# Attention tiles: rows and keys turned head by head, gate logits summed in PSUM, and the scalar and vector steps in a new order

## The chip, the core and the metric

The kernel runs on one core of a Trainium2 chip. The metric is the device time of one execution in microseconds. PE is TensorE (PEld its weight loads), DVE is VectorE, ACT ScalarE, POOL GpSimd, SP SyncE. A tile here is 128 tokens; a tile's index is written t, and its place in its batch c = t mod 6.

## What is computed

The reference has three stages. The change touches the first one and its handover to the second.

```python
def _attn_ref(q, k, v, f_logit):          # 4 batches, 8 heads, 768 tokens, 48 channels a head
    f = 1.0 / (1.0 + np.exp(-f_logit))
    for t in range(S):
        state = f[:, :, t, :, None] * state + np.einsum('bhd,bhe->bhde', k[:, :, t], v[:, :, t])
        y[:, :, t] = np.einsum('bhd,bhde->bhe', q[:, :, t], state)
# x = y by token: 3072 x 384; logits = x @ w_gate (8 experts)
# _moe_ref: (token, expert) pairs in falling order of logits, each expert takes N/8 = 384 tokens;
#           out[mask] = relu(x[mask] @ w1[e]) @ w2[e]
# _moe2_ref: g = elu(x @ w_in); g @ w_out
```

## The kernel before

`attention` goes through 24 tiles, six to a batch. Four pairs of heads lie side by side; of a pair one head's 48 channels are on partitions 0 to 47, the other's on 64 to 111 (`par` 0 and 1), so a [P, pairs, P] buffer is 128 x 512. Decays become products along the tokens: `growth` is 1 + exp(-f), `rb` is its running product (scans on DVE, L522), `guess` is exp(-ln rb), and one Newton step makes of it `nb`, minus the reciprocal (`near` on DVE at L504, `gap`, `nb` and `q_s` on POOL at L318, L324 and L330). k_s = k * rb (L529).

On PE each tile has six groups. `turned_keys` (L623) turns k_s by a full-width transpose for each of the 4 pairs; `scores` (L637) makes 8 products k_s by q_s into two banks `a_ps[0]` and `a_ps[1]`; DVE masks them with `causal` (L492, one instruction a bank); `from_state` (L594) and `from_tile` (L604) add the carried state's and the tile's own part into `y_ps`; `state_parts` (L613) makes k_tok by v into `ds_ps`, which DVE turns into the new `state` (L481 subtract, L483 multiply); `turned` (L580) multiplies the finished columns `x_tr` by `turn_gate`, identity and gate weights beside each other, and so gives rows and, for each pair apart, gate logits. Tiles with c = 0 need no `from_state` products and no subtraction, tiles with c = 5 no keys turned and no state.

The order of the work is written out by hand: `run_steps` gives every engine a `step` s, in which tiles of several ages are served, and each engine's queue is in order. In step s:

- PE (L641): turned(s-5), from_state(s-4), from_tile(s-4), state_parts(s-4), turned_keys(s-2), scores(s-3).
- DVE (L495): near(s-2), scan(s-1), k_s(s-1), subtract and multiply of the state (s-4), both masks (s-3).
- ACT (L382): e_x(s), gate and row copies (s-5, L367 and L368), x_tr(s-4, L376), the row store, k_tok(s-2, L404), Ln(s-1, L412), ends(s-1, L413), growth(s, L419), Exp(s-1, L423).
- POOL (L310): gap, nb and q_s of s-2.

`from_tile` waits for both masks of its tile (`am_ready`, L600), `scores` for both masks of the tile before (L632), `from_state` for the state of the tile before (L588). Behind the loop POOL adds the gate parts of the first 20 tiles (L348 to L351), DVE those of the last four (L565), and the search for the experts' tokens starts (`begin_tiles`, L83, and `search` in `route_and_feed`).

Of the kernel before, what the change touches and what calls it, by code (L numbers as in the profile page):

```python
# [36 lines left out]
def program(nc, q_t, k_t, f_t, v_rows, q_heads, k_heads, f_heads, v_heads, w_gate, gate_rows, w1, w2, w_in, w_out, out):  # L37
# [3 lines left out]
    with ExitStack() as ctx:  # L41
# [20 lines left out]
        def sem(name):  # L62
# [9 lines left out]
        hit_ready = sem("hit_ready")  # L72
        block = ctx.enter_context(nc.Block())
        flag = {}
        attention(nc, block, sem, q_t, k_t, f_t, v_rows, w_gate, w_in, w_out, x_dram, w_in_raw, w_in_hi, w_out_raw, logits, x_row, x_stored,
                  ident, w_in_loaded, w_out_loaded, w_in_upper, overflow, over_known, logits_ready, consts, scan, open_step, hit_ready, flag)
# [3 lines left out]
                       x_row, x_stored, consts, scan, open_step, hit_ready, out)  # L80
# [23 lines left out]
def attention(nc, block, sem, q_t, k_t, f_t, v_rows, w_gate, w_in, w_out, x_dram, w_in_raw, w_in_hi, w_out_raw, logits, x_row, x_stored, ident,  # L104
              w_in_loaded, w_out_loaded, w_in_upper, overflow, over_known, logits_ready, consts, scan, open_step, hit_ready, flag):
# [13 lines left out]
    HALF = 64  # L119
    PR = HALF + dim  # L120
# [3 lines left out]
    with ExitStack() as ctx:  # L124
# [18 lines left out]
        k_tok = [sb(f"k_tok{i}", [P, pairs, P]) for i in range(2)]  # L143
# [49 lines left out]
        x_ready = sem("x_ready")  # L193
# [31 lines left out]
        def carried(b, c, plus=0):  # L225

            at_c = c + plus
            if at_c < 0:
                return b * CARRY + min(at_c + 1, 0)
            return b * CARRY + min(at_c + 1, CARRY)  # L230

        @block.sync
        def _(sp):
# [31 lines left out]
            for c in range(2, per_batch):  # L265
# [22 lines left out]
        def _(pool):  # L288
# [9 lines left out]
            for i in range(2, 6):  # L298
# [50 lines left out]
            nc.gpsimd.tensor_tensor(gate_parts[:, early, 2, :], gate_parts[:, early, 2, :], gate_parts[:, early, 3, :], ALU.add).then_inc(logits_begun, 1)  # L349
            pool.wait_ge(logits_begun, 2)  # L350
            nc.gpsimd.tensor_tensor(logits[:, early, :], gate_parts[:, early, 0, :], gate_parts[:, early, 2, :], ALU.add).then_inc(logits_begun, 1)  # L351

        @block.scalar
        def _(act):
# [6 lines left out]
            def row_parts(pb, c, bank, reused):  # L361

                act.wait_ge(xr_done, number(pb, c, 1, 1))
# [3 lines left out]
                nc.scalar.copy(gate_parts[:, bass.ds(pb * per_batch + c, 1), :, :], bank[:, :, PR:PR + experts].unsqueeze(1)).then_inc(gate_read, 1)  # L367
# [14 lines left out]
            def step(o, b, s):  # L382
# [1386 lines left out]
```

## Time and profile before

| | us |
|---|---|
| median of 3 runs | 856.01 (855.54 to 856.14) |
| the profiled execution | 854.62, its span 852.7 |
| attention, first scores to last scores | 14.67 to 128.02 |
| PE busy over the span | 790.8 (93%) |
| DVE, ACT, POOL busy over the span | 493.7 (58%), 465.6 (55%), 528.3 (62%) |

The page's averages are mostly those of the expert stages behind 175 us. The attention stage has its own limits, to be read from the stretch 60 to 120 us and from the timeline of a single tile. A timeline row gives start and length; where instructions of one line follow each other they are merged, and the length is that of the whole piece. "Idle before" in brackets is how long the engine stood still before the piece and what ended that.

### The profile page before, as it was taken

The numbers are of one execution on the slowest core, as the hardware profiler recorded it, in microseconds if no ns is written. First come the engines' busy times: TensorE is split into PE (matmuls) and PEld (weight loads), VectorE is DVE, ScalarE is ACT, GpSimd is POOL, SyncE is SP. The second block draws the span as 40 slices with busy tenths as digits, with TensorE's granted clock in tenths as the row PEclk, the third lists the DMA queues.
The fourth block names the chain that finished last, engine by engine and source line by source line (L and its number), as shares of the span: only waits on it lengthen the run. The fifth ranks groups of instructions, "written<-read, shape, count | busy, mean of one in ns | idle before, by whom it ended". The sixth has DMA issues, their size and how long they took to land.

```text
span 852.7 us, 19225 instructions
## 1 busy us (share of the span) xinstructions
PE 790.8 (93%) x6378; PEld 748.9 (88%) x6378; DVE 493.7 (58%) x994; ACT 465.6 (55%) x980; POOL 528.3 (62%) x500
## 2 busy tenths in 40 slices
PE   3999995489999999999999999999999999999995
PEld 2888884378889899989988999899989999999995
DVE  6899998884784476448635764486448426430001
ACT  5677756142664277418732774187428744863653
POOL 8788884477784278527842785278518763964562
PEclk9999997599999999999999999999999999999999
DMA  7777690500410041004100410040004004100000
GB/s 194 208 207 205 195 366 35 184 2 2 148 30 8 23 149 29 13 17 150 28 10 25 148 29 11 19 150 28 20 10 153 25 29 148 28 2 29 1 1 28
DMA packets 33751, 65.83 MB, mean 77 GB/s; under 512 B 4560, under 2 KB 20944, under 8 KB 33280
## 3 DMA queue, kind: packets, MB, share of 16 engines
q1 hardware_dynamic: 27072, 50.36, 18.2%
q0 software_dynamic: 3136, 9.64, 3.5%
q10 hardware_dynamic: 3456, 4.72, 1.6%
q8 instruction: 49, 0.80, 0.4%
q14 instruction: 38, 0.31, 0.1%
HBM read 55.26 MB, written 9.44 MB: 76 GB/s over the span
## 4 chain that ended last, share of the span: by engine, by line
PE 80%; POOL 5%; issue 4%; DVE 4%; ACT 3%; DMA 1%; ACTq 0%; POOLq 0%; SPq 0%; DVEq 0%
PE o_ps L1420 8%; PE o_ps L1421 7%; PE o_ps L1422 7%; PE m_ps L1408 7%; PE m_ps L1409 6%; PE m_ps L1404 6%; PE m_ps L1360 4%; PE o_ps L1378 4%; PE m_ps L1358 4%; PE m_ps L1361 4%; PE o_ps L1380 3%; PE o_ps L1379 3%; PE a_ps L637 3%; PE y_ps L604 3%; PE r_ps L1277 2%
## 5 line engine op out<-in xcount | busy, mean ns | idle before, releaser
L1074 POOL TENSOR_TENSOR t_lo<-whole,t_hi 128x384 fp32r<-128x384 f32 x190 | 203.4, 1072 | 100.1 <-ACT t_hi L1155 98.4
L1102 POOL TENSOR_TENSOR whole<-whole,below 128x384 f32<-128x384 f32 x126 | 133.1, 1057 | 154.2 <-ACT below L1174 153.3
L1408 PE MATMUL m_ps<-y_hi,w_in_hi 128*128 128x384 f32 x384 | 134.4, 350 | 4.3 <-ACT y_hi L1186 4.3
L1420 PE MATMUL o_ps<-w_out_hi,t_hi 128*128 128x384 f32 x378 | 129.7, 343 | 3.4 <-POOL t_lo L1074 2.4
L1409 PE MATMUL m_ps<-y_hi,w_in_low 128*128 128x384 f32 x384 | 129.6, 338 | 0.0
L1421 PE MATMUL o_ps<-w_out_low,t_hi 128*128 128x384 f32 x378 | 127.5, 337 | 0.0
L1422 PE MATMUL o_ps<-w_out_hi,t_lo 128*128 128x384 f32 x378 | 127.1, 336 | 0.0
L1170 ACT ACTIVATE whole<-m_ps 128x384 f32<-128x384 f32 x128 | 62.8, 490 | 93.5 <-PE m_ps L1404 87.3
L1154 ACT ACTIVATE whole<-m_ps 128x384 f32<-128x384 f32 x64 | 31.5, 492 | 130.4 <-PE m_ps L1358 121.0
L1404 PE MATMUL m_ps<-y_lo,w_in_hi 128*128 128x384 f32 x384 | 87.0, 338 | 0.0
L1408 PEld LDWEIGHTS m_ps<-y_hi,w_in_hi 128*128 128x128 f32 x384 | 72.3, 188 | 6.4 <-issue 6.4
L1420 PEld LDWEIGHTS o_ps<-w_out_hi,t_hi 128*128 128x128 f32 x378 | 71.3, 189 | 6.7 <-issue 6.6
L1174 ACT ACTIVATE below<-below 128x384 f32<-128x384 f32 x128 | 67.3, 526 | 16.3
L1409 PEld LDWEIGHTS m_ps<-y_hi,w_in_low 128*128 128x128 f32 x384 | 72.4, 189 | 0.0
L1421 PEld LDWEIGHTS o_ps<-w_out_low,t_hi 128*128 128x128 f32 x378 | 71.2, 188 | 0.0
L1422 PEld LDWEIGHTS o_ps<-w_out_hi,t_lo 128*128 128x128 f32 x378 | 71.2, 188 | 0.0
L1162 ACT CAST t_hi<-whole 128x384 fp32r<-128x384 f32 x128 | 64.0, 500 | 13.1 <-POOL whole L1102 12.0
L1404 PEld LDWEIGHTS m_ps<-y_lo,w_in_hi 128*128 128x128 f32 x384 | 68.9, 189 | 0.0
L1378 PE MATMUL o_ps<-t_hi,w_hi 128*128 128x384 f32 x192 | 67.8, 353 | 1.1 <-POOL t_lo L1074 1.1
L1360 PE MATMUL m_ps<-x_hi,w_hi 128*128 128x384 f32 x192 | 66.4, 346 | 2.1 <-ACT x_hi L1204 1.5
L1380 PE MATMUL o_ps<-t_lo,w_hi 128*128 128x384 f32 x192 | 64.6, 337 | 0.0
L1379 PE MATMUL o_ps<-t_hi,w_low 128*128 128x384 f32 x192 | 64.6, 336 | 0.0
(236 smaller groups left out, 1690.7 us busy)
## 6 DMA issues: line engine op xcount, KB each, us to landing
w_raw<-w SPq DMA_DIRECT2D x16, 1536.0 KB, 7.8
f_in<-f_t SPq DMA_DIRECT2D x48, 96.0 KB, 2.5
k_in<-k_t SPq DMA_DIRECT2D x48, 96.0 KB, 2.6
q_in<-q_t SPq DMA_DIRECT2D x48, 96.0 KB, 2.5
v_in<-v_rows SPq DMA_DIRECT2D x24, 192.0 KB, 2.8
x_scratch<-x_row ACTq DMA_DIRECT2D x24, 192.0 KB, 2.5
w_in_raw<-w_in SPq DMA_DIRECT2D x1, 3072.0 KB, 11.6
w_out_raw<-w_out SPq DMA_DIRECT2D x1, 3072.0 KB, 20.8
```

What stands on the lines that cost most here:

```text
L1074: nc.gpsimd.tensor_tensor(t_lo[n % RING][:], whole[n % 3][:], t_hi[n % RING][:], ALU.subtract).then_inc(lo_made, 1)
L1102: nc.gpsimd.tensor_tensor(tile[:], tile[:], below[m % 2][:], ALU.subtract).then_inc(g_made, 1)
L1360: nc.tensor.matmul(m_ps[m % RING][:], w1_hi[:, t, cols], x_hi[:, t, :], start=(t == 0), stop=False)
L1378: nc.tensor.matmul(o_ps[j][:], w2_hi[:, m, cols], hi[:], start=(m == 0), stop=False)
L1379: nc.tensor.matmul(o_ps[j][:], w2_low[:, m, cols], hi[:], start=False, stop=False)
L1380: ins = nc.tensor.matmul(o_ps[j][:], w2_hi[:, m, cols], lo[:], start=False, stop=(m == MH - 1))
L1404: ins = nc.tensor.matmul(bank[:], w_in_hi[:, t, cols], y_lo[:, t, :], start=False, stop=(t == KD - 1))
L1408: nc.tensor.matmul(bank[:], w_in_hi[:, t, cols], y_hi[:, t, :], start=(t == 0), stop=False)
L1409: nc.tensor.matmul(bank[:], w_in_low[:, t, cols], y_hi[:, t, :], start=False, stop=False)
L1420: nc.tensor.matmul(o_ps[t][:], hi[:, rows], w_out_hi[:, m, :], start=(m == 0), stop=False)
L1421: nc.tensor.matmul(o_ps[t][:], hi[:, rows], w_out_low[:, m, :], start=False, stop=False)
L1422: ins = nc.tensor.matmul(o_ps[t][:], lo[:, rows], w_out_hi[:, m, :], start=False, stop=(m == MI - 1))
```

## The change

- The full-width transposes of the keys become two for each pair, one a head (48 partitions), and so do the rows: instead of the product with `turn_gate`, 8 transposes of 48 partitions, by single-pass transposes. Keys, rows and the gate logits lie in one pair of banks, `turn_ps`, so `turned` waits for the copy of the keys (`ktok_ready`), and `turned_keys` for the copy of the rows (`x_ready`).
- The gate logits are four products added up in PSUM (`gates_of`), which ACT copies straight into `logits`. The sums on POOL and DVE go; POOL's `turn_gate` is now a small zeroed `gate_in`.
- ACT's Ln waits for the scan, not for k_s, and Exp comes ahead of growth.
- DVE's step becomes: scan(s-1), state subtract(s-4), mask of `par` 0 (s-3), k_s(s-1), near(s-1), state multiply(s-4), mask of `par` 1 (s-3). near is made a step earlier. k_s waits for `ends`.
- The last two tiles' gates are turned into spare places ahead of their rows, and the search waits for the row copies only in its second round.

PE's step order and the waits of `from_state`, `from_tile`, `state_parts` and `scores` are as before.

```diff
-kt_ps = ps("kt_ps", [P, pairs, P])
-a_ps = [ps(f"a_ps{i}", [P, pairs, P]) for i in range(2)]
+a_ps = ps("a_ps", [P, 2, BANK])
 y_ps = ps("y_ps", [P, pairs, P])
 ds_ps = ps("ds_ps", [P, pairs, dim])
-xr_ps = ps("xr_ps", [P, pairs, P])
+turn_ps = ps("turn_ps", [P, 2, BANK])
+HALF_ROW = pairs * dim
+kt_ps = turn_ps[:, :, 0:HALF_ROW]
+turned_rows = turn_ps[:, :, HALF_ROW:2 * HALF_ROW]
+turned_gates = turn_ps[:, 0, 2 * HALF_ROW:2 * HALF_ROW + experts]
+spare_rows = a_ps[:, :, 0:HALF_ROW]
+spare_gates = [rb[:, 0, 0:experts], growth[:, 0, 0:experts]]
...
-        return b * CARRY + min(at_c + 1, 0)
+        return b * CARRY + min(at_c + 2, 0)
...
-            nc.gpsimd.tensor_copy(turn_gate[0:PR, :, 0:PR], ident[0:PR, 0:PR].unsqueeze(1).to_broadcast([PR, pairs, PR])).then_inc(zeros_ready, 1)
+            nc.gpsimd.memset(gate_in[:], 0.0).then_inc(zeros_ready, 1)
...
-    pool.wait_ge(x_ready, EARLY)
-    pool.sem_inc(nb_turn, 1)
-    early = slice(0, EARLY)
-    nc.gpsimd.tensor_tensor(gate_parts[:, early, 0, :], gate_parts[:, early, 0, :], gate_parts[:, early, 1, :], ALU.add).then_inc(logits_begun, 1)
...
-    def row_parts(pb, c, bank, reused):
+    def gate_part(pb, c, gates):
+        nc.scalar.copy(logits[:, bass.ds(pb * per_batch + c, 1), :], gates.unsqueeze(1)).then_inc(gate_read, 1)
+    def row_part(pb, c, rows, reused):
         act.wait_ge(xr_done, number(pb, c, 1, 1))
         if reused:
             act.wait_ge(x_stored[c % 3], pb * 32 + ((c // 3) * 16 + 1))
-        nc.scalar.copy(gate_parts[:, bass.ds(pb * per_batch + c, 1), :, :], bank[:, :, PR:PR + experts].unsqueeze(1)).then_inc(gate_read, 1)
-        nc.scalar.copy(x_row[c % 3][:].rearrange("p (j u d) -> p j u d", u=2, d=dim),
-                       bank[:].rearrange("p j (u d) -> p j u d", u=2)[:, :, :, 0:dim]).then_inc(x_ready, 1)
+            act.sem_inc(row_turn, 1)
+        nc.scalar.copy(x_row[c % 3][:].rearrange("p (j u d) -> p u j d", u=2, d=dim), rows.rearrange("p u (j d) -> p u j d", d=dim)).then_inc(x_ready, 1)
...
-            nc.scalar.copy(k_tok[c % 2][:, :, 0:PR], kt_ps[:, :, 0:PR]).then_inc(ktok_ready, 1)
+            nc.scalar.copy(k_tok[c % 2][:], kt_ps).then_inc(ktok_ready, 1)
         if 1 <= s <= tiles:
             pb, c = at(b, o, 1)
-            act.wait_ge(k_ready, number(pb, c, 1, 1))
+            act.wait_ge(rbeta_ready, number(pb, c, 1, 1))
             if s >= 3:
                 act.wait_ge(beta_ready, number(pb, c, 1, -1))
             nc.scalar.activation(guess[c % 2][:], rb[:], ACT.Ln).then_inc(ln_ready, 1)
             nc.scalar.copy(ends[:, bass.ds(pb * per_batch + c, 1), :], rb[:, :, P - 1:P].rearrange("p a b -> p b a")).then_inc(end_ready, 1)
-        if s < tiles:
-            act.wait_ge(exp_ready, number(b, o, 1, 1))
-            if s >= 1:
-                act.wait_ge(rbeta_ready, number(b, o))
-            nc.scalar.activation(growth[:], e_x[o % 2][:], ACT.Identity, bias=1.0).then_inc(growth_ready, 1)
         if 1 <= s <= tiles:
             pb, c = at(b, o, 1)
             act.wait_ge(ln_ready, number(pb, c, 1, 1))
             nc.scalar.activation(guess[c % 2][:], guess[c % 2][:], ACT.Exp, scale=-1.0).then_inc(guess_ready, 1)
+        if s < tiles:
+            act.wait_ge(exp_ready, number(b, o, 1, 1))
+            if s >= 1:
+                act.wait_ge(rbeta_ready, number(b, o))
+            nc.scalar.activation(growth[:], e_x[o % 2][:], ACT.Identity, bias=1.0).then_inc(growth_ready, 1)
...
+    for i in range(2):
+        act.wait_ge(gates_done, i + 1)
+        act.sem_inc(row_turn, 1)
+        gate_part(end, 4 + i, spare_gates[i])
+    row_part(end, 4, spare_rows, True)
+    row_part(end, 5, turned_rows, True)
...
+    def state_less(pb, c):
+        dve.wait_ge(ds_done, carried(pb, c))
+        if c > 0:
+            dve.wait_ge(state_ready, carried(pb, c, -1))
+            nc.vector.tensor_tensor(ds_ps[0:PR], ds_ps[0:PR], state[0:PR], ALU.subtract).then_inc(state_sum, 1)
     def carry_state(pb, c, first):
         end = nb[c % 3][0:PR, :, P - 1:P].to_broadcast([PR, pairs, dim])
-        dve.wait_ge(ds_done, carried(pb, c))
         dve.wait_ge(beta_ready, number(pb, c, 1, 1))
         if not first:
             dve.wait_ge(state_ready, carried(pb, c, -1))
         if c > 0:
-            nc.vector.tensor_tensor(ds_ps[0:PR], ds_ps[0:PR], s_ap, ALU.subtract).then_inc(state_sum, 1)
             dve.wait_ge(state_sum, pb * (CARRY - 1) + c)
-        nc.vector.tensor_tensor(s_ap, ds_ps[0:PR], end, ALU.mult).then_inc(state_ready, 1)
-    def mask_scores(b, o, s):
+        nc.vector.tensor_tensor(state[0:PR], ds_ps[0:PR], end, ALU.mult).then_inc(state_ready, 1)
+    def mask_scores(b, o, s, par):
         pb, c = at(b, o, 3)
-        for par in range(2):
-            dve.wait_ge(a_done, number(pb, c, 2, 2))
-            if s >= 5 and par == 0:
-                dve.wait_ge(y_made, number(pb, c, 1, -1))
-            nc.vector.tensor_tensor(a_m[c % 2][:, par], a_ps[par][:],
-                                    causal[:].unsqueeze(1).to_broadcast([P, pairs, P]), ALU.mult).then_inc(am_ready, 1)
+        dve.wait_ge(a_done, number(pb, c, 2, 1 + par))
+        if s >= 5 and par == 0:
+            dve.wait_ge(y_made, number(pb, c, 1, -1))
+        nc.vector.tensor_tensor(a_m[c % 2][:, par], a_ps[:, par].rearrange("p (j t) -> p j t", j=pairs),
+                                causal[:].unsqueeze(1).to_broadcast([P, pairs, P]), ALU.mult).then_inc(am_ready, 1)
     def step(o, b, s):
-        if 2 <= s <= tiles + 1:
-            pb, c = at(b, o, 2)
-            dve.wait_ge(guess_ready, number(pb, c, 1, 1))
-            dve.wait_ge(end_ready, number(pb, c, 1, 1))
-            if s >= 4:
-                dve.wait_ge(beta_ready, number(pb, c, 1, -1))
-            nc.vector.tensor_tensor(near[c % 2][:], rb[:], guess[c % 2][:], ALU.mult).then_inc(near_ready, 1)
...
+        hands_on = 4 <= s and (o - 4) % per_batch < CARRY
         if 1 <= s <= tiles:
             pb, c = at(b, o, 1)
...
-            dve.wait_ge(rbeta_ready, number(pb, c, 1, 1))
-            dve.wait_ge(k_loaded[c], pb * K_LOADED + K_LOADED)
-            if s >= 4:
-                dve.wait_ge(a_done, number(pb, c, 2, -4))
-            nc.vector.tensor_tensor(k_s[c % 3][:], k_in[c][:], rb[:], ALU.mult).then_inc(k_ready, 1)
-        if 4 <= s and (o - 4) % per_batch < CARRY:
-            pb, c = at(b, o, 4)
-            carry_state(pb, c, s == 4)
...
+        if hands_on:
+            state_less(*at(b, o, 4))
         if s == tiles + 2:
+            carry_state(*at(b, o, 4), False)
...
-            mask_scores(b, o, s)
+            mask_scores(b, o, s, 0)
+        if 1 <= s <= tiles:
+            pb, c = at(b, o, 1)
+            dve.wait_ge(rbeta_ready, number(pb, c, 1, 1))
+            dve.wait_ge(end_ready, number(pb, c, 1, 1))
+            dve.wait_ge(k_loaded[c], pb * K_LOADED + K_LOADED)
+            if s >= 4:
+                dve.wait_ge(a_done, number(pb, c, 2, -4))
+            nc.vector.tensor_tensor(k_s[c % 3][:], k_in[c][:], rb[:], ALU.mult).then_inc(k_ready, 1)
+        if 1 <= s <= tiles:
+            pb, c = at(b, o, 1)
+            dve.wait_ge(guess_ready, number(pb, c, 1, 1))
+            if s >= 3:
+                dve.wait_ge(beta_ready, number(pb, c, 1, -1))
+            nc.vector.tensor_tensor(near[c % 2][:], rb[:], guess[c % 2][:], ALU.mult).then_inc(near_ready, 1)
+        if hands_on and s < tiles + 2:
+            carry_state(*at(b, o, 4), s == 4)
+        if 3 <= s:
+            mask_scores(b, o, s, 1)
...
-    dve.wait_ge(logits_begun, 3)
-    early, rest = slice(0, EARLY), slice(EARLY, tiles)
+    dve.wait_ge(triangle, 4)
+    dve.wait_ge(gate_read, EARLY)
...
-    dve.wait_ge(x_ready, tiles - 1)
     dve.wait_ge(gate_read, tiles)
-    then(v.tensor_reduce(logits[:, rest], gate_parts[:, rest].rearrange("p t j e -> p t e j"), AX.X, ALU.add))
...
-    def turned(pb, c, bank, start, reused):
+    def gates_of(c, gates):
+        for j in range(pairs):
+            ins = nc.tensor.matmul(gates, x_tr[c % 2][0:PR, j, :], gate_in[0:PR, j, :], start=(j == 0), stop=(j == pairs - 1))
+        return ins
+    def rows_of(c, rows):
+        for j in range(pairs):
+            for par in range(2):
+                at_head = slice(par * HALF, par * HALF + dim)
+                ins = nc.tensor.transpose(rows[:, par, j * dim:(j + 1) * dim], x_tr[c % 2][at_head, j, :], ident[at_head, at_head])
+        return ins
+    def turned(pb, c, start, reused, keys_read):
         pe.wait_ge(xt_ready, number(pb, c, 1, 1))
         if start:
             pe.wait_ge(gate_loaded, 32)
         if reused is not None:
             pe.wait_ge(x_ready, reused)
-        for j in range(pairs):
-            ins = nc.tensor.matmul(bank[:, j, 0:PR + experts], x_tr[c % 2][0:PR, j, :], turn_gate[0:PR, j, :], start=True, stop=True)
-        ins.then_inc(xr_done, 1)
+        pe.wait_ge(ktok_ready, keys_read)
+        pe.sem_inc(a_turn, 1)
+        gates_of(c, turned_gates)
+        rows_of(c, turned_rows).then_inc(xr_done, 1)
...
-    def turned_keys(pb, c, first):
+    def turned_keys(pb, c, first, rows_read):
         pe.wait_ge(k_ready, number(pb, c, 1, 1))
         if not first:
             pe.wait_ge(ktok_ready, carried(pb, c, -1))
+        if rows_read is not None:
+            pe.wait_ge(x_ready, rows_read)
+        pe.sem_inc(a_turn, 1)
         for j in range(pairs):
-            ins = nc.tensor.transpose(kt_ps[:, j, 0:PR], k_s[c % 3][0:PR, j, :], ident[0:PR, 0:PR])
+            for par in range(2):
+                rows = slice(par * HALF, par * HALF + dim)
+                ins = nc.tensor.transpose(kt_ps[:, par, j * dim:(j + 1) * dim], k_s[c % 3][rows, j, :], ident[rows, rows])
...
-            turned(pb, c, xr_ps, s == 5, number(pb, c) if s >= 6 else None)
+            kb, kc = at(b, o, 3)
+            turned(pb, c, s == 5, number(pb, c) if s >= 6 else None, carried(kb, kc))
...
+    pe.wait_ge(xt_ready, number(end, 4, 1, 1))
+    pe.wait_ge(near_ready, tiles)
+    pe.sem_inc(a_turn, 1)
+    gates_of(4, spare_gates[0]).then_inc(gates_done, 1)
+    rows_of(4, spare_rows).then_inc(xr_done, 1)
+    pe.wait_ge(xt_ready, number(end, 5, 1, 1))
     pe.wait_ge(rbeta_ready, tiles)
-    turned(end, 4, growth, False, None)
-    turned(end, 5, xr_ps, False, number(end, 4))
+    pe.sem_inc(a_turn, 1)
+    gates_of(5, spare_gates[1]).then_inc(gates_done, 1)
+    pe.wait_ge(x_ready, number(end, 4))
+    pe.sem_inc(a_turn, 1)
+    rows_of(5, turned_rows).then_inc(xr_done, 1)
...
-OPENED = 7
+OPENED = 6
...
+            if fresh and i == 1:
+                dve.wait_ge(x_ready, tiles)
```

## Rows read from the trace of the kernel before

**Rows 1.** Busy time by stretch: from:to, length, each engine (instructions), granted clock, DMA.

```profile
60.00:120.00 60.00, 59.17 (x878) 51.85 (x876) 54.64 (x119) 44.24 (x107) 50.23 (x38) 1.00 0.75 235
```

**Rows 2.** Chain that ended last: the score matmuls of two tiles, six tiles apart.

```profile
66.35 1.09 PE a_ps L637 x16
...
95.43 1.09 PE a_ps L637 x16
```

**Rows 3.** Timeline, TensorE, one tile: start, length, engine, line, operation.

```profile
85.72 1.16 PE L637 MATMUL a_ps<-q_s,k_s 48*128 48x128 f32 x16
...
86.81 0.97 PEld L580 LDWEIGHTS xr_ps<-turn_gate,x_tr 112*128 112x128 f32 x8
...
86.82 1.15 PE L580 MATMUL xr_ps<-turn_gate,x_tr 112*128 112x120 f32 x8
...
87.90 1.08 PE L594 MATMUL y_ps<-q_s,state 48*48 48x128 f32 x16
...
88.91 1.08 PE L604 MATMUL y_ps<-a_m,v_in 128*48 128x128 f32 x16
...
89.82 0.53 PE L613 MATMUL ds_ps<-v_in,k_tok 128*48 128x48 f32 x16
...
90.28 0.60 PE L623 MATMUL kt_ps<-ident,k_s 112*128 112x112 f32 x4
...
90.81 1.16 PE L637 MATMUL a_ps<-q_s,k_s 48*128 48x128 f32 x16
```

**Rows 4.** Timeline, VectorE, the same tile.

```profile
85.54 0.69 DVE L529 TENSOR_TENSOR k_s<-k_in,rb 128x512 f32<-128x512 f32 x1
...
86.14 0.36 DVE L481 TENSOR_TENSOR ds_ps<-ds_ps,state 112x192 f32<-112x192 f32 x1
...
86.54 0.36 DVE L483 TENSOR_TENSOR state<-ds_ps,nb 112x192 f32<-112x192 f32 x1
...
86.96 1.29 DVE L492 TENSOR_TENSOR a_m<-a_ps,causal 128x512 f32<-128x512 f32 x2
...
88.17 0.68 DVE L504 TENSOR_TENSOR near<-rb,guess 128x512 f32<-128x512 f32 x1
...
88.95 1.38 DVE L522 TENSOR_TENSOR_SCAN rb<-growth,growth_cap 128x128 f32<-128x128 f32 x4
```

**Rows 5.** Timeline, ScalarE and GpSimd, the same tile.

```profile
85.83 0.53 ACT L404 COPY k_tok<-kt_ps 128x448 f32<-128x448 f32 x1 [0.29 <-PE kt_ps L623]
...
86.26 0.60 ACT L412 ACTIVATE guess<-rb 128x512 f32<-128x512 f32 x1
...
86.75 0.16 ACT L413 COPY ends<-rb 128x4 f32 x1
...
87.33 0.64 ACT L423 ACTIVATE guess<-guess 128x512 f32<-128x512 f32 x1
...
89.04 1.49 POOL L318 TENSOR_SCALAR near<-near 128x512 f32<-128x512 f32 x1 [0.54 <-DVE near L504]
...
92.31 1.28 POOL L330 TENSOR_TENSOR q_s<-q_in,nb 128x512 f32<-128x512 f32 x1 [0.33 <-POOL nb L324]
```

**Rows 6.** Timeline, TensorE, while the pipeline fills.

```profile
13.04 0.98 PE L623 MATMUL kt_ps<-ident,k_s 112*128 112x112 f32 x4 [4.26 <-ACT k_tok L404]
...
14.67 2.08 PE L637 MATMUL a_ps<-q_s,k_s 48*128 48x128 f32 x16 [0.65 <-POOL q_s L330]
...
22.18 1.47 PE L637 MATMUL a_ps<-q_s,k_s 48*128 48x128 f32 x16
```

**Rows 7.** Timeline, TensorE and VectorE, the last tile and the routing's start.

```profile
128.02 1.16 PE L637 MATMUL a_ps<-q_s,k_s 48*128 48x128 f32 x16
...
135.23 0.38 DVE L565 TENSOR_REDUCE logits<-gate_parts 128x32 f32<-128x128 f32 x1
...
136.07 0.19 DVE L88 TENSOR_REDUCE best<-logits 128x4 f32<-128x32 f32 x1 [0.46 <-DVE logits L565]
```

**Rows 8.** Busy time by stretch, behind attention; columns as in Rows 1.

```profile
134.00:138.00 4.00, 1.21 (x26) 0.97 (x25) 3.21 (x8) 3.26 (x5) 0.00 (x0) 1.00 0.27 100
```

More of the change, by code:

```diff
@@ L119, in attention @@
     HALF = 64
+    BANK = 512
     PR = HALF + dim
@@ L142, in attention @@
         k_s = [sb(f"k_s{i}", [P, pairs, P]) for i in range(3)]
-        k_tok = [sb(f"k_tok{i}", [P, pairs, P]) for i in range(2)]
+        k_tok = [sb(f"k_tok{i}", [P, 2, pairs * dim]) for i in range(2)]
         a_m = [sb(f"a_m{i}", [P, 2, pairs, P]) for i in range(2)]
@@ L419, in step @@
                     nc.scalar.activation(growth[:], e_x[o % 2][:], ACT.Identity, bias=1.0).then_inc(growth_ready, 1)
-                if 1 <= s <= tiles:
-                    pb, c = at(b, o, 1)
-                    act.wait_ge(ln_ready, number(pb, c, 1, 1))
-                    nc.scalar.activation(guess[c % 2][:], guess[c % 2][:], ACT.Exp, scale=-1.0).then_inc(guess_ready, 1)
             run_steps(act, step, tiles + 2)
@@ L523, in step @@
                     ins.then_inc(rbeta_ready, 1)
-                    dve.wait_ge(rbeta_ready, number(pb, c, 1, 1))
-                    dve.wait_ge(k_loaded[c], pb * K_LOADED + K_LOADED)
-                    if s >= 4:
-                        dve.wait_ge(a_done, number(pb, c, 2, -4))
-                    nc.vector.tensor_tensor(k_s[c % 3][:], k_in[c][:], rb[:], ALU.mult).then_inc(k_ready, 1)
-                if 4 <= s and (o - 4) % per_batch < CARRY:
-                    pb, c = at(b, o, 4)
-                    carry_state(pb, c, s == 4)
+                if s == tiles + 1:
+                    c = (o - 2) % per_batch
+                    dve.wait_ge(near_ready, tiles)
+                    dve.wait_ge(beta_ready, tiles - 1)
+                    dve.wait_ge(state_ready, carried(batches - 1, c, -3))
+                    nc.vector.scalar_tensor_tensor(out=nb[c % 3][:], in0=near[c % 2][:], scalar=-2.0, in1=guess[c % 2][:],
+                                                   op0=ALU.add, op1=ALU.mult).then_inc(beta_ready, 1)
+                    dve.wait_ge(beta_ready, tiles)
+                    dve.wait_ge(y_made, tiles - 3)
+                    dve.wait_ge(q_ready, tiles - 1)
+                    dve.wait_ge(qv_loaded[c], batches * QV_LOADED)
+                    nc.vector.tensor_tensor(q_s[c % 3][:], q_in[c][:], nb[c % 3][:], ALU.mult).then_inc(q_ready, 1)
+                if hands_on:
+                    state_less(*at(b, o, 4))
                 if s == tiles + 2:
+                    carry_state(*at(b, o, 4), False)
                     tables()
@@ L636, in scores @@
                         rows = slice(par * HALF, par * HALF + dim)
-                        ins = nc.tensor.matmul(a_ps[par][:, j, :], k_s[c % 3][rows, j, :], q_s[c % 3][rows, j, :], start=True, stop=True)
+                        ins = nc.tensor.matmul(a_ps[:, par, j * P:(j + 1) * P], k_s[c % 3][rows, j, :], q_s[c % 3][rows, j, :], start=True, stop=True)
                         if j == pairs - 1:
@@ L816, in route_and_feed @@
 def route_and_feed(nc, block, sem, w1, w2, x_dram, w_in_raw, w_in_low, w_in_hi, w_in_upper, w_out_raw, w_out_low, logits, ident, w_out_loaded,
-                   x_row, x_stored, consts, scan, open_step, hit_ready, out):
+                   x_row, x_stored, consts, scan, open_step, hit_ready, x_ready, out):
     experts, width, hidden = w1.shape
```

62 lines of the change are left out of this document (26 added, 36 removed).

## The prediction

> **What bounds the kernel now.** I read the busy time by stretch first, because the page's averages belong to the expert stages. From 60 to 120 us PE is busy for 59.17 of 60 us and DVE for 54.64; ACT and POOL have room [rows 1]. The chain of waits says the same: it runs through PE groups without a break, and two scores six tiles apart stand 29.08 us apart, 4.85 us a tile [rows 2]. The timeline of one tile then shows what those are [rows 3]: scores start at 85.72, turned at 86.82, from_state at 87.90, from_tile at 88.91, state_parts at 89.82, turned_keys at 90.28, the next scores at 90.81. The start-to-start spacings are 1.10 + 1.08 + 1.01 + 0.91 + 0.46 + 0.53 = 5.09 us: PE's own work, end to end.
>
> The second thing to read is a loop that lies just below this. Scores start at 85.72, the masks at 86.96, and both masks end at 88.25 [rows 3, 4]. from_tile could start then, but PE is still in from_state and starts it at 88.91: 0.66 us of slack. So the loop scores, masks, from_tile, state_parts, keys, scores is worth 5.09 - 0.66 = 4.43 us, and PE's throughput (5.09) hides it. Every tile closes this loop once: scores(t+1) waits for both masks of t, and from_tile(t) stands ahead of it in PE's queue and waits for them too. What lengthens it by more than 0.66 us sets the pace.
>
> **The change part by part.** The profiled execution took 854.62 us, its span 852.7; the median of the runs is 856.01, so 1.39 more. I sum against 854.62 and add 1.39 at the end.
>
> *The split masks and DVE's new order.* This is the term that counts. DVE's spacings in the tile shown [rows 4]: k_s to the subtraction 0.60 (85.54 to 86.14), subtraction to multiplication 0.40, multiplication to masks 0.42, a mask 0.60 (half of 86.96 to 88.17), near to scan 0.78, of which the scan waits for near. In the new order the first mask is followed by k_s, near and the state's multiplication, and only then comes the second mask. I count from the start of scores(t), taking 0.60 for a mask, k_s and near each (near was not seen before an independent instruction; 0.60 is k_s's value, 0.78 the upper end):
>
> - first mask at 1.24 (86.96 - 85.72, the same wait as now); k_s at 1.84; near at 2.44; multiplication of state t-1 at 3.04, done at 3.40 (0.36 long).
> - from_state(t) waits for this state. With 0.08 from an end to the start it releases (scores end at 85.72 + 1.16 = 86.88, masks start at 86.96) it starts at 3.48. The second mask starts at 3.46 and ends at 4.15.
> - from_tile at 3.48 + 1.01 = 4.49 (the second mask is done by then, 0.34 to spare), state_parts at 5.40, turned_keys at 5.86, and scores(t+1) at 5.86 plus the keys' new cost.
>
> So near and k_s, 1.20 us that now run before or after the loop, lie inside it, and from_state (1.01), which now runs beside the masks, lies behind the new state. Nothing on PE is left to run in the gap but turned.
>
> *The keys' transposes* (L623): 4 of 112 partitions and 112 columns take 0.53 from start to start, 133 ns each [rows 3]. They become 8 of 48 partitions, 128 columns loaded and 48 streamed. No row shows this form. The bounds come from the nearest two-by-two groups: state_parts, 16 instructions of 48 columns in 0.46, is 29 ns each, so 0.23; without any overlap of the two heads 8 x 133 ns are 1.06. Scores, also on 48 partitions with 128 columns loaded, take 1.09 for 16, 68 ns, with 128 columns streamed; that is the nearest row, and as fewer columns are streamed here I take 46 ns, 0.37 in all. The loop's step is then 5.86 + 0.37 = 6.23 us.
>
> The Trainium skill ("TensorE: Matmul & The Clock Gate", section "LDWEIGHTS (loading the stationary operand)") says that a weight load takes as long as its columns, however few its rows, about 107 ns for 128 columns. By this the keys would take 0.85, and the sum below would be some 9 us higher. The scores rows at 68 ns for the same 128 columns disagree, as long as the two heads overlap.
>
> *The other tiles of a batch.* c = 0 has no from_state products and no multiplication: second mask 3.04 to 3.73, from_tile 3.81, scores 5.55. c = 3 has no keys in its step (those of c = 5 are not turned): 5.86. c = 5 has no state_parts: 5.77. c = 1, 2, 4: 6.23. A batch takes 5.55 + 3 x 6.23 + 5.86 + 5.77 = 35.87 us where it took 29.08 [rows 2]: 1.13 more a tile.
>
> *Over the stage.* Scores of tile 1 start at 22.18 [rows 6] and of tile 23 at 128.02 [rows 7]: 105.84 for 22 steps. New: tiles 1 to 5 30.32, two batches 71.74, tiles 18 to 21 23.87, and tile 22, whose masks have no k_s and near between them, 1.24 + 0.60 + 0.36 + 0.08 + 1.01 + 0.46 + 1.01 = 4.76. The sum is 130.69, so 24.85 more. The keys' bounds, in 18 of these steps, shift it by -2.5 and +12.4; near at 0.78 by +3.6.
>
> *Rows and gates* (L580, 1.08 from start to start). The 8 transposes cost what the keys' do, 0.37 (0.23 to 1.06). The gates are the same 8 weight loads with 8 columns streamed instead of 120: at most the present 1.08, at least 8 x 29 ns = 0.23; I take the loads' own 0.97 [rows 3]. turned is 1.34, between 0.46 and 2.14. It starts with the end of scores, at 1.10, and from_state cannot start before 3.48, so 2.38 us are free for it even at its upper bound: nothing. Were PE the limit, it would cost 0.26 a tile. PE's whole work would be 5.09 - 0.16 + 0.26 = 5.19: no relief there anyway.
>
> *The new waits.* turned waits for the copy of the keys, which starts 0.11 behind scores' start and takes 0.53 [rows 5]: done before scores end. turned_keys waits for the rows' copy, about 2 us earlier in its step than the keys: free. k_s waits for ends, near for Exp. In the new loop ACT is held in its queue by the keys' copy: it ends about 0.6 into the next step, Ln (0.60) then runs to 1.2, ends to 1.3, Exp to 1.9 (lengths in [rows 5]), against k_s at 1.84 and near at 2.44. Both are covered by about 0.5. If keys take their upper bound this cover goes down to nothing, but then the step is longer as well. The subtraction of the state runs before the first mask, while DVE has nothing to do: free. POOL needs 5.42 us from near to the end of q_s (88.17 to 93.59, [rows 4, 5]) and now has more than a step and a half.
>
> *Start.* The first scores stand behind keys whose place in PE's queue waits for the first copy of keys (4.26 us idle, [rows 6]); POOL's shorter setup changes nothing there. Between the first two scores (at the low clock) the split masks add about 0.7 and the keys take 0.3 off: +0.4.
>
> *End.* POOL's sums are hidden now. DVE's sum of the last gates goes with the wait behind it: 135.23 to 136.07 [rows 7], -0.84. The stages behind start later and are otherwise the same.
>
> Sum: 24.85 + 0.4 - 0.84 = 24.4. 854.62 + 24.4 = 879.0 for an execution like the profiled one, and 880.4 for the median.
>
> **The rivals.**
>
> - *TensorE's clock falls in the new waits.* PE would be idle for about 1.05 us of each 6.23. At the first scores the group takes 2.08 instead of 1.16 [rows 6]: that is 1.2 against 2.4 GHz. PE's part of the loop, 1.16 + 1.01 + 0.91 + 0.46 + 0.37 = 3.91 us, would double. With a quarter of the 22 steps at 1.2 GHz this is +21, so 901. Against it: behind attention PE is busy for 1.21 of 4 us and the granted clock still is 1.00 [rows 8]. By the Trainium skill (the same page, "Part 4: PE-mode transpose") transposes do not count as TensorE activity in the way that products do, and the change has more of them; the keys' rows here, between products, show the full clock. Chance 0.10.
> - *A smaller loss.* Half of the 1.13 a tile shows, because a link is shorter than counted, as where masks release earlier or DVE's spacings shrink: 854.62 + 12 + 1.39 = 868. Chance 0.07.
> - *Faster: PE's throughput stays the bound.* This decides if the loop stays below 5.09, so if it lost 1.14 us of what I count. Then the keys (-0.16 in 18 steps) and turned at a gate cost half of the loads' (-0.23 in 22) give -8, and the end -0.8, less what DVE (54.64 of 60 busy) then limits: -6 to -7, 849. It needs k_s and near not to stand between the masks, which the code contradicts. Chance 0.05.
> - *Nothing moves.* The order costs nothing and PE's work stays as it is (5.19 against 5.09, above, with the end's gain): 856. Chance 0.04.
>
> **How the numbers follow.** The forecast, 880.4, has the rest, 0.74, with a range of its own from 874 to 894 by the keys' and near's bounds. The range, 867 to 898, takes in the smaller loss and leaves out the slow clock's centre, the faster and the unchanged case, about 0.2. Faster by over 0.2% (1.7 us, about what a measurement can tell from no change) has 0.05, within it 0.04, slower 0.91.
>
> **What would show it.** Right: scores of c = 1 and 2 about 6.2 us apart; PE idle between turned and from_state for some 1 us, released by the state's multiplication (state, L483 before); DVE idle before its first mask, released by scores; PE busy well below 59 of 60 us. Wrong: scores 5.1 or less apart, or ACT (Ln, Exp) or the keys' copy named as what PE or DVE waits for. The prediction fails most easily at the cost of the small transposes, and if something in the stage lets the second mask come earlier than the queue's order says.

## The result and the profile after

| | before | after |
|---|---|---|
| median, us | 856.08 (855.54 to 857.53, 4 runs) | 916.41 (906.25 to 919.34, 4 runs) |
| profiled execution, its span | 854.62, 852.7 | 919.34, 917.5 |
| scores of tile 1 to scores of tile 23 | 22.18 to 128.02, 4.81 a tile | 21.82 to 195.53, 7.90 a tile |
| from there to the last `begin_tiles` | 8.05 | 8.26 |

The ratio is 1.068 (1.064 to 1.072): 60 us slower, where 24 were forecast. All of it lies in the attention stage: between the two profiles the stage is 67.9 us longer and the span 64.8, since the part behind the last scores is 2.7 shorter. The page shows where to look, in the rows for PE and for its clock (busy share and granted clock in tenths, 40 slices of the span; the last line is the clock's row of the kernel before):

```profile
PE   3989899982899899999999999999999999999996
...
PEclk9876767675899999999999999999999999999998
...
PEclk9999997599999999999999999999999999999999
```

Attention fills the first six slices before and the first eight and a half after. There the clock's row had 9 throughout and now reads 6 to 8 behind its first slice; the 5 behind the stage stands in both. Busy time by stretch (length, then busy us and instructions of PE, PEld, DVE, ACT, POOL, the granted clock, the DMA share, GB/s) says how much, for the stretch of [rows 1] and for two short ones inside it:

```profile
60.00:120.00 60.00, 53.72 (x611) 48.22 (x608) 30.47 (x69) 29.34 (x69) 30.77 (x24) 0.67 0.44 126
...
86.70:90.20 3.50, 2.53 (x40) 2.26 (x36) 2.54 (x6) 3.11 (x8) 0.13 (x1) 0.92 0.70 202
90.20:94.40 4.20, 4.17 (x46) 3.82 (x48) 1.81 (x5) 0.30 (x1) 3.88 (x3) 0.50 0.22 66
```

PE is busy for 53.72 of 60 us, but the granted clock is 0.67, and it changes within a single tile: 0.92, then 0.50. PE's timeline of this tile (start, length, engine, line, operation) shows what comes before the fall; the first row is from the tile before it:

```profile
82.47 1.68 PE L626 MATMUL y_ps<-q_s,state 48*48 48x128 f32 x16 [0.96 <-DVE state L493]
...
86.74 1.13 PE L674 MATMUL a_ps<-q_s,k_s 48*128 48x128 f32 x16
...
87.79 1.06 PE L592 MATMUL turn_ps<-gate_in,x_tr 112*128 112x8 f32 x8
...
88.78 0.45 PE L601 MATMUL turn_ps<-ident,x_tr 48*128 48x48 f32 x8
...
90.23 1.95 PE L626 MATMUL y_ps<-q_s,state 48*48 48x128 f32 x16 [1.01 <-issue]
...
92.11 1.95 PE L636 MATMUL y_ps<-a_m,v_in 128*48 128x128 f32 x16
...
94.63 2.02 PE L674 MATMUL a_ps<-q_s,k_s 48*128 48x128 f32 x16
```

Scores, gates and row transposes run at 2.4 GHz. Then PE waits for 1.01 us (in the tile before for 0.96, and there the state is named as what ended the wait), and from_state takes 1.95 us where it took 1.08 [rows 3], from_tile 1.95, the next scores 2.02: 1.2 GHz. VectorE's rows of the same stretch are the new order:

```profile
87.98 0.69 DVE L501 TENSOR_TENSOR a_m<-a_ps,causal 128x512 f32<-128x512 f32 x1 [0.96 <-PE a_ps L674]
...
88.59 0.68 DVE L545 TENSOR_TENSOR k_s<-k_in,rb 128x512 f32<-128x512 f32 x1
...
89.18 0.69 DVE L553 TENSOR_TENSOR near<-rb,guess 128x512 f32<-128x512 f32 x1
...
89.78 0.35 DVE L493 TENSOR_TENSOR state<-ds_ps,nb 112x192 f32<-112x192 f32 x1
90.05 0.68 DVE L501 TENSOR_TENSOR a_m<-a_ps,causal 128x512 f32<-128x512 f32 x1
```

The first mask starts 1.24 behind scores (86.74), the state's multiplication at 3.04, from_state at 3.49. These are the forecast's numbers (1.24, 3.04, 3.48). What follows on PE, up to and with the next scores, has the lengths of half the clock; the gates behind them are back at 1.06 us.

### The profile page after: what moved, and what is told of

Read it like the earlier page. It is cut to its first block, busy times and chain, and to the rows that moved or that the text cites. A ratio compares the mean times of both kernels' runs of the same rounds, so it can differ in the third digit from the quotient of the medians.

```text
span 917.5 us, 19859 instructions
## 1 busy us (share of the span) xinstructions
PE 840.4 (92%) x6650; PEld 796.9 (87%) x6650; DVE 486.3 (53%) x993; ACT 467.1 (51%) x980; POOL 525.5 (57%) x496
## 4 chain that ended last, share of the span: by engine, by line
PE 79%; issue 6%; POOL 5%; DVE 3%; ACT 3%; DMA 1%; ACTq 0%; SPq 0%; DVEq 0%; POOLq 0%
PE o_ps L1467 7%; PE o_ps L1469 7%; PE o_ps L1468 7%; PE m_ps L1455 6%; PE m_ps L1456 6%; PE m_ps L1451 6%; PE y_ps L636 5%; PE y_ps L626 4%; PE m_ps L1407 4%; PE o_ps L1425 3%; PE m_ps L1405 3%; PE m_ps L1408 3%; PE a_ps L674 3%; PE o_ps L1427 3%; PE o_ps L1426 3%
## 5 line engine op out<-in xcount | busy, mean ns | idle before, releaser
L321 POOL TENSOR_SCALAR near<-near 128x512 f32<-128x512 f32 x23 | 34.3, 1489 | 74.6 <-DVE near L553 74.6
```

## The experiments

Theory A: the new order opens a loop of about 6.2 us a tile; the wait that it leaves on PE lets the clock fall, and this doubles PE's part of the loop. Rivals: the small transposes and gate products cost the time whatever the order; or the order costs nothing. Four kernels tell these apart.

**The old order with the new transposes** (e1). In the changed kernel, DVE's and ACT's steps are those of before. The lines on DVE's and ACT's steps, here and below, give their order in short and are not code.

```diff
 # DVE, one step
-scan(s-1); state_less(s-4); mask(s-3, 0); k_s(s-1); near(s-1); carry_state(s-4); mask(s-3, 1)
+near(s-2); scan(s-1); k_s(s-1); state_less(s-4); carry_state(s-4); mask(s-3, 0); mask(s-3, 1)
 # ACT
-Ln waits for rbeta_ready; Exp; growth
+Ln waits for k_ready; growth; Exp
```

> The changed kernel with the old order on VectorE and ScalarE (near of s-2 first, then scan, k_s, state, both masks side by side; Ln behind k_s, growth ahead of Exp); transposes, gates and banks stay new. Theory A (the order alone opened a loop of 6.2 us, and the waits it leaves on TensorE let its clock fall): PE is dense again at 1.10 + 0.99 + 0.41 + 1.01 + 0.91 + 0.46 + 0.29 = 5.17 us a tile against 5.09 before, granted clock about 1.00 in the stage, median 856 to 858. Theory B (the small transposes and the gate products keep TensorE's clock low whatever the order): granted clock about 0.7 in the stage and over 890.

Measured: 855.16 (852.36 to 856.93), ratio 0.9995 (0.9973 to 1.0017). The clock from 60 to 120 us:

```profile
60.00:120.00 60.00, 59.90 (x1002) 54.47 (x1000) 54.80 (x119) 45.03 (x111) 50.14 (x39) 1.00 0.72 218
```

The whole loss is gone (the median is 0.8 us under the range); the transposes and gates alone take none of the time. PE's groups add up to 5.08 us where keys are turned (scores at 88.94 and 94.02), not less than before, so the head by head transposes bring nothing here either. In its profile the stage is 4.4 us longer than before (tiles 1 to 23 from 21.16 to 131.41), but 3.8 us of this lie between tiles 1 and 2, 9.23 us apart where they were 5.39, with groups as long as at the low clock (scores of tile 1 take 2.04 us).

**The new order with the old transposes** (e2), in the kernel before.

```diff
 # DVE, one step, and ACT's order the other way round
-near(s-2); scan(s-1); k_s(s-1); state subtract, multiply(s-4); mask(s-3, 0); mask(s-3, 1)
+scan(s-1); state subtract(s-4); mask(s-3, 0); k_s(s-1); near(s-1); state multiply(s-4); mask(s-3, 1)
```

> The kernel before with only the new order on VectorE and ScalarE and the split masks; TensorE's groups, banks and gate sums are the old ones. Theory A1 (idle alone lets the clock fall): the wait before from_state is about 1.3 us (2.38 less the 1.08 of turned), granted clock about 0.7 in the stage, 910 or more. Theory A2 (it takes the wait together with the new weight-heavy groups in front of it): granted clock near 1.00, a step of 6.2 + 0.24 (keys at 0.53 instead of 0.29) = 6.4 us and about 856 + 22 x 1.3 = 885. Theory B: the same as A2 in the clock. If the order is not the cause: 856.

Measured: 885.71 (884.03 to 889.77), ratio 1.037 (1.032 to 1.041). It is A2's 885. The clock (busy time by stretch), and PE's timeline, the last row from a tile with c = 0:

```profile
60.00:120.00 60.00, 47.88 (x671) 41.67 (x669) 40.28 (x90) 36.13 (x87) 38.12 (x29) 0.97 0.52 156
```

```profile
85.19 1.16 PE L649 MATMUL a_ps<-q_s,k_s 48*128 48x128 f32 x16
86.28 1.15 PE L592 MATMUL xr_ps<-turn_gate,x_tr 112*128 112x120 f32 x8
88.64 1.08 PE L606 MATMUL y_ps<-q_s,state 48*48 48x128 f32 x16 [1.20 <-issue]
89.65 1.08 PE L616 MATMUL y_ps<-a_m,v_in 128*48 128x128 f32 x16
...
95.00 1.44 PE L616 MATMUL y_ps<-a_m,v_in 128*48 128x128 f32 x16 [1.57 <-DVE a_m L495]
```

The wait ahead of from_state (L606) is 1.20 us, longer than the changed kernel's 1.01, and from_state still takes 1.08. So the order alone costs 31 us against the 854.55 of the kernel before measured beside it, most of it through the loop, with the clock at 0.97. Behind the old product of 1.15 us a wait of 1.20 us doesn't lower the clock, but a longer one can: tiles with c = 0 wait for 1.57 us ahead of from_tile, and in two of three such tiles the groups behind it were slow (1.44 us at 95.00 and 1.95 at 133.27, but 1.08 at 58.27). So theory A1, that idle time alone does it, is wrong for the waits of most tiles here and not for all waits.

**The wait filled** (e3): four products into `y_ps`, which from_state overwrites.

```diff
                     pe.wait_ge(xt_ready, number(pb, c))
+                    if c > 0:
+                        pe.sem_inc(a_turn, 1)
+                        for _ in range(4):
+                            nc.tensor.matmul(y_ps[:, 0, :], ident[:], causal[:], start=True, stop=True, skip_group_check=True)
                     pe.wait_ge(state_ready, carried(pb, c, -1))
```

> The changed kernel with four additional full-width products (identity by mask, some 1.08 us at the full clock) in TensorE's queue just ahead of from_state's wait for the state; their output is overwritten. Theory A: the wait is filled, the granted clock is back at 1.00 and the loop shows at its bare length of 6.1 to 6.3 us for tiles 1, 2 and 4 of a batch: median 876 to 884, in spite of 18 to 20 us of additional TensorE work. Theory B (the time goes to TensorE's work, not to its clock): slower than the changed kernel, 920 or more.

Measured: 887.40 (886.04 to 894.63), ratio 1.040 (1.034 to 1.046). More work on PE makes the changed kernel 29 us faster: it wasn't PE's work that took the time. The median is 3 us above what A said. The clock is 0.91 from 60 to 120 us. Tiles with c = 0 have no additional products and still wait for 1.21 us, and behind two of these three waits the groups are slow, up to the next tile's scores and beyond:

```profile
94.04 1.08 PE L640 MATMUL y_ps<-a_m,v_in 128*48 128x128 f32 x16 [1.21 <-DVE a_m L501]
...
96.16 2.04 PE L678 MATMUL a_ps<-q_s,k_s 48*128 48x128 f32 x16
```

**Gates streamed wider** (e5). e2 differs from the changed kernel in what PE does ahead of the wait. This run changes that alone: the gate products stream 120 columns, 112 of them zeros, instead of 8 (those of the last two tiles stay as they are).

```diff
-gate_in = sb("gate_in", [P, pairs, experts])
+gate_in = sb("gate_in", [P, pairs, 120])
...
+wide_gates = turn_ps[:, 0, 2 * HALF_ROW:2 * HALF_ROW + 120]
...
 # in turned()
-gates_of(c, turned_gates)
+gates_of(c, wide_gates)
```

> The changed kernel; only the gate products stream 120 columns (112 of them zeros) instead of 8 into the same bank, as the old product did. Their time should not move, since the eight loads (0.97 us) bound them already (1.06 against 1.15 us). Theory A2 (the clock falls because a wait of 1 us follows 1.4 us of groups that load weights and stream nearly nothing): granted clock over 0.95 in the stage, the loop at its bare 6.2 us, median 878 to 888. Rival A3 (the eight transposes and the wait are enough by themselves): clock stays near 0.7, 905 to 920.

Measured: 878.50 (876.72 to 880.06), ratio 1.026 (1.023 to 1.029). Busy time by stretch, and PE's timeline:

```profile
60.00:120.00 60.00, 51.08 (x841) 45.26 (x840) 43.49 (x99) 37.41 (x90) 40.33 (x30) 1.00 0.60 167
```

```profile
82.02 1.12 PE L675 MATMUL a_ps<-q_s,k_s 48*128 48x128 f32 x16
83.07 1.15 PE L593 MATMUL turn_ps<-gate_in,x_tr 112*128 112x120 f32 x8
84.15 0.45 PE L602 MATMUL turn_ps<-ident,x_tr 48*128 48x48 f32 x8
85.43 1.08 PE L627 MATMUL y_ps<-q_s,state 48*48 48x128 f32 x16 [0.83 <-issue]
86.44 1.08 PE L637 MATMUL y_ps<-a_m,v_in 128*48 128x128 f32 x16
```

The gates take 1.15 instead of 1.06 us, the wait is 0.83, and the clock is 1.00 throughout. That the wait is 0.18 us shorter is not what keeps the clock: in the tile with c = 0 PE waits for 1.12 us (ahead of from_tile at 91.51) and the groups behind keep their lengths. 37.9 us of the loss (916.41 - 878.50) are the clock's, and what is left, 23 us, is the loop by itself: scores of tile 1 at 22.12 and of tile 23 at 151.04, 128.92 us for the 22 steps.

**Which half of the order costs the loop.** Three arrangements of VectorE's step in the changed kernel; in e4 both masks and the state come ahead of k_s and near, in e7 the masks only, in e8 the state only.

```diff
-scan; state_less; mask 0; k_s; near; carry_state; mask 1
+scan; state_less; carry_state; mask 0; mask 1; k_s; near     # e4
+scan; state_less; mask 0; mask 1; k_s; near; carry_state     # e7
+scan; state_less; carry_state; mask 0; k_s; near; mask 1     # e8
```

> The changed kernel with VectorE's step turned: scan, state subtract, state multiply, both masks side by side, then k_s and near. Ln still waits for the scan. Theory A: k_s and near are out of the loop between scores and from_tile, which falls back to about 4.4 us, so PE's 5.17 us a tile set the pace: 855 to 859 at a granted clock of 1.00. Rival: what costs is that near is made in the same step as its scan, so VectorE waits for Ln and Exp (about 1.4 us behind the scan): 870 or more, with near waiting for guess.

> The changed kernel with both masks side by side ahead of k_s and near, the state's multiplication last. It separates the two halves of the new order: here the masks are together, but from_state waits for a state that comes behind k_s and near. Theory A: the step at the full clock is 1.24 + 1.20 + 1.20 + 0.36 + 0.08 + 1.01 + 0.91 + 0.46 + 0.29 = 6.75 us, longer than the changed kernel's 6.15; TensorE waits some 1.6 us a tile and its clock falls as there: 920 to 945. Rival (it is the split of the masks that costs): 855 to 870.

> The changed kernel with the state's multiplication moved ahead of the first mask; the masks stay apart, with k_s and near between them. Theory A: from_state is free again, the second mask ends at 3.73 us behind scores' start and the step is 3.81 + 0.91 + 0.46 + 0.29 = 5.47 us, 0.30 over TensorE's own 5.17; TensorE waits only 0.3 us a tile, so the clock stays at 1.00: 858 to 864. Rival (split masks are the larger half): 875 or more.

Measured: e4 854.81 (851.48 to 860.20), ratio 0.9997 (0.9971 to 1.0024); e7 913.20 (909.29 to 914.32), 1.065 (1.061 to 1.069); e8 871.28 (867.25 to 875.57), 1.018 (1.014 to 1.023). One step of e7, with both masks together:

```profile
81.43 1.12 PE L673 MATMUL a_ps<-q_s,k_s 48*128 48x128 f32 x16
...
82.58 1.29 DVE L501 TENSOR_TENSOR a_m<-a_ps,causal 128x512 f32<-128x512 f32 x2 [0.96 <-PE a_ps L673]
...
83.79 0.68 DVE L546 TENSOR_TENSOR k_s<-k_in,rb 128x512 f32<-128x512 f32 x1
...
84.38 0.68 DVE L554 TENSOR_TENSOR near<-rb,guess 128x512 f32<-128x512 f32 x1
...
84.98 0.35 DVE L493 TENSOR_TENSOR state<-ds_ps,nb 112x192 f32<-112x192 f32 x1
...
85.48 1.08 PE L625 MATMUL y_ps<-q_s,state 48*48 48x128 f32 x16 [1.56 <-DVE state L493]
...
88.14 1.13 PE L673 MATMUL a_ps<-q_s,k_s 48*128 48x128 f32 x16
```

From scores to scores it is 6.71 us (81.43 to 88.14, forecast 6.75), all at the full clock, and from_state waits 1.56 us for the state. The wait of the next tile is as long and leaves the clock as well; the one after it doesn't:

```profile
92.23 1.08 PE L625 MATMUL y_ps<-q_s,state 48*48 48x128 f32 x16 [1.60 <-issue]
...
98.65 1.94 PE L625 MATMUL y_ps<-q_s,state 48*48 48x128 f32 x16 [1.51 <-issue]
```

So the split of the masks isn't the main cost; the state's multiplication behind k_s and near is. e8 confirms the smaller half: in its profile the steps of tiles with keys are 5.35 to 5.43 us where the clock holds (5.43 from 81.71 to 87.14), where 5.47 was worked out. Two totals were off. e7 came out 7 us below its range, because its clock is 0.77 and not lower than the changed kernel's 0.67, in spite of the longer wait. e8 is 7 us above its range: its clock is 0.96 from 20 to 60 us and 0.94 from 100 to 120, and two of its three waits of 1.2 us ahead of from_tile where c = 0 are followed by slow groups (the next scores take 1.89 and 1.73 us). Some 3 us of it lie elsewhere: in its profile the part behind the last scores is 727.6 us, 724.7 before. Why the longer waits of e7 lower the clock less stays open, and so does what decides for one tile: the same groups and the same wait are followed by either clock. e4, 0.2 us under its range, also answers its rival: near in the same step as its scan costs nothing that the time shows once ACT's Ln comes straight behind the scan.

**A version that beats both** (e6). With the order of e4, PE's own groups set the pace, and these can be chosen apart. The keys' transposes fell to 0.29 us from 0.53; gates and rows rose to 1.37 (0.99 and 0.38) from 1.08. So e6 keeps the one and takes back the other.

```diff
 # order of e4; keys head by head
-gates_of(c, turned_gates)
-rows_of(c, turned_rows).then_inc(xr_done, 1)
+for j in range(pairs):     # two pairs to a bank of turn_ps, behind the keys' columns
+    ins = nc.tensor.matmul(turned_all[:, j // 2, j % 2, 0:PR + experts], x_tr[c % 2][0:PR, j, :], turn_gate[0:PR, j, :], start=True, stop=True)
+ins.then_inc(xr_done, 1)
 # gate sums on POOL and DVE as in the kernel before
```

> The order of e4 (scan, state, both masks, then k_s and near) and the keys turned head by head, but rows and gates by the old product of 1.08 us, two pairs to a bank, with the gate sums on GpSimd and VectorE as in the kernel before. Theory A (TensorE's groups set the pace once the order is right): 1.10 + 1.08 + 1.01 + 0.91 + 0.46 + 0.29 = 4.85 us a tile instead of 5.17 in e4 and 5.09 before, VectorE's own 4.83 just below; 849 to 852, ratio to the kernel before 0.992 to 0.996. Rival (VectorE or ScalarE, with one more copy a tile, now ends last): 854 to 856, no difference.

Measured: 850.20 (847.99 to 850.65), ratio 0.9919 (0.9894 to 0.9944). The chosen step, from scores to scores:

```profile
85.11 1.12 PE L663 MATMUL a_ps<-q_s,k_s 48*128 48x128 f32 x16
...
89.90 1.12 PE L663 MATMUL a_ps<-q_s,k_s 48*128 48x128 f32 x16
...
20.73 2.04 PE L663 MATMUL a_ps<-q_s,k_s 48*128 48x128 f32 x16
...
29.55 1.39 PE L663 MATMUL a_ps<-q_s,k_s 48*128 48x128 f32 x16
```

It is 4.79 us, forecast 4.85. The second pair of rows is from the fill: scores of tiles 1 and 2 stand 8.82 us apart, with the first at 2.04 us, the length of the low clock.

**Products while the pipeline fills** (e9), in e6: 7 of them ahead of the first keys, 10 ahead of the second.

> e6 with 7 additional full products on TensorE ahead of the first keys and 10 more ahead of the second keys, while the pipeline fills; their output is overwritten. In e6's profile the groups run at the low clock until 30 us (scores of 2.07 and 2.04, from_state and from_tile of 1.95 us), and its scores of tiles 1 and 2 stand 8.8 us apart where 4.8 is the steady step. Theory (this part of the fill is the clock's): the first groups take about half, tiles 1 and 2 are 5 us apart, and the median falls by 4 to 6 us against e6's 850.2, to 844 to 847 (ratio to the kernel before 0.986 to 0.990). Rival (the fill waits for the loads and VectorE, the clock only shows): 849 to 852.

Measured: 847.72 (846.92 to 853.24), ratio 0.9913 (0.9886 to 0.9940).

```profile
18.79 1.16 PE L672 MATMUL a_ps<-q_s,k_s 48*128 48x128 f32 x16
...
23.92 1.15 PE L672 MATMUL a_ps<-q_s,k_s 48*128 48x128 f32 x16
```

The fill is as worked out: 5.13 us between these scores, at 1.16 and 1.15 us each, and the last scores start at 120.00 instead of 125.89. The median fell by 2.5 us and not by 4 to 6, and the two intervals overlap, so a gain over e6 is not shown by the times; the part behind the last scores was 725.1 us in this profile, 722.9 in e6's. Nor is it shown that e6's fill is slow each time, since each kernel has one profile: the kernel before and e4 have 5.39 and 5.26 us between these scores without additional products.

## Why the prediction was wrong

**The loop was right**, in place and in size. From the profile of e5, where it shows at the full clock: tile steps (scores at 63.92 to 99.24) of 6.12, 5.87, 6.11, 5.72, 5.43 and 6.07 us from scores to scores against 6.23, 5.86, 6.23, 5.77, 5.55 and 6.23 worked out. The sum for 22 steps was 130.69, measured 128.92. The difference lies mainly in the keys' term: taken at 0.37, it measured 0.29 from start to start, between that and its lower bound of 0.23. e5's median, 878.5, lies 1.9 from the forecast 880.4. As one kernel's result this is the forecast; but the changed kernel is not e5.

**The step that failed is the clock's.** It stood as a rival with 0.10 and +21 us for a quarter of the steps. Against e5 it measured 44.8 us in the stage (173.71 against 128.92; this profile is the slowest of the four executions) and 37.9 in the medians. By the prediction's own price, 3.91 us a slow step, 44.8 are 11.5 of the 22 steps: not only the chance but also the quarter was too low. Two readings led there.

- [Rows 8] were taken as evidence that waits don't lower the clock: PE busy for 1.21 of 4 us, and 1.00. That stretch lies directly behind a dense one. The next four microseconds of the same trace, in which PE is busy for about as long, were left out of the account:

```profile
138.00:142.00 4.00, 1.35 (x30) 1.13 (x30) 2.51 (x10) 4.00 (x3) 1.35 (x3) 0.61 0.02 4
```

- turned's change was costed by its time alone, 1.34 us against 1.08, and called free because the wait behind it covers it. The time was right (1.37) and it was covered. But the group also changed in kind: products that stream 120 columns became products that stream 8, and transposes of 48. e5 shows that the gates' 8 columns alone, with the transposes kept, were worth 37.9 us, in a place that costs no time by itself. The Trainium skill's sentence that transposes don't count as TensorE activity in the way that products do ("TensorE: Matmul & The Clock Gate", "Part 4: PE-mode transpose") was cited and set aside with rows in which the keys stand between dense products. e1 agrees with these rows (clock 1.00 with all the new groups, PE dense); e5 adds that the same transposes with a wait behind them keep 1.00 as well, once the gates are wide. What lowers the clock in the changed kernel is the narrow gates together with the wait; no run here has these two without the row transposes, so whether the transposes have a share stays open.

**The small terms.** The end was to give 0.84; from the last scores to the last `begin_tiles` it is 7.94 us in e1 against 8.05 before, 0.1. DVE's sum went, but DVE then waits for the last tile's gates, 0.62 us in e1:

```profile
138.75 0.17 ACT L359 COPY logits<-growth 128x8 f32<-128x8 f32 x1 [1.20 <-PE growth L585]
...
139.35 0.19 DVE L89 TENSOR_REDUCE best<-logits 128x4 f32<-128x32 f32 x1 [0.62 <-ACT logits L359]
```

The start was to cost 0.4. The first two scores stand 7.64 us apart, 7.51 before, so it cost 0.1; with the first of them earlier, at 14.18, scores of tile 1 start at 21.82, 0.4 earlier than before [rows 6]. The new waits (keys' copy, rows' copy, ends, Exp) appear in no row of the waits between 60 and 110 us of the changed kernel, as worked out. Weight loads for the small transposes: the keys came to 36 ns each, so the 46 ns taken, scaled down from scores' 68, were too high. The Trainium skill's rule of 107 ns for 128 columns ("TensorE: Matmul & The Clock Gate", "LDWEIGHTS (loading the stationary operand)") doesn't describe these pairs; the measured rows decide.

**The rivals.** The forecast's own range is added up wrongly: 880.4 with the keys' bounds (-2.5, +12.4) and near's (+3.6) gives 878 to 896, not 874 to 894. This decides nothing here. "Nothing moves" is what e1 shows for the new transposes alone, by a balance the prediction had: PE's work is the same. "Faster" needed what e6 does: another order, and only the keys' transposes. The range of 867 to 898 left out the slow clock by counting it as one case of ten beside the loop, when in this kernel the loop brought it on: the forecast itself put a wait of 1 us into every step, behind groups that it had made narrow.

## What to carry to other kernels

When a change leaves a wait on TensorE in every step, cost the clock as part of the forecast and not as an accident beside it, and read what stands ahead of the wait: here two groups of the same length, one streaming 8 columns and one 120, differed by 38 us in what the clock did behind them. When an in-order queue is rearranged, follow every result that another engine returns to the same loop; an instruction put ahead of such a result (here k_s and near ahead of the state) costs its full length in each turn, even on an engine that is busy for half of the time. Where weight loads bound a product, streaming zeros beside the useful columns cost 0.09 us a group here and kept the clock. What decides for a single tile is not known from these runs, so such a change has to be measured.

## What the runs showed of the hardware

- Eight transposes of 48 partitions, two heads in turn into two banks, take 0.29 us from start to start, 36 ns each; four of 112 partitions took 0.53.
- A product that loads 128 columns of fp32 weights for 8 streamed ones takes nearly the time of its loads (0.97 us): 0.99 us for eight passes, where 120 streamed columns take 1.08.
- The granted clock fell within a tile, from 0.92 to 0.50, behind gates, transposes and 1.01 us of waiting; behind the old product and 1.20 us it stayed. It is no fixed rule: behind the old product and 1.57 us it fell in two tiles of three (e2), and behind narrow gates and waits of 1.56 and 1.60 us it stayed in at least two tiles of e7, whose mean is 0.77.
- Products that nobody reads made a kernel faster: e3 by 29 us. Those of e9 shortened its fill, but its median doesn't show a gain.
- In the fill of e6 the groups have the lengths of 1.2 GHz while no lower clock is shown in the clock's column; there the column doesn't show what the lengths do:

```profile
20.00:30.00 10.00, 10.00 (x101) 8.96 (x99) 5.21 (x13) 4.43 (x12) 7.10 (x6) 1.00 0.62 191
```
